# A fused attention, dense and expert kernel: TensorE's order inside an expert tile

## The reference

```python
# x: 3072 x 512 (output of the dense layer), w1: 8 x 512 x 1024, w2: 8 x 1024 x 512
logits = x @ w_gate
expert_idx = np.argmax(logits, axis=1)
probs = softmax(logits)
gate_w = probs[np.arange(N), expert_idx]
for e in range(8):
    mask = expert_idx == e
    h = np.maximum(x[mask] @ w1[e], 0.0)
    out[mask] = gate_w[mask, None] * (h @ w2[e])
```

## Time and profile before

| | |
|---|---|
| median of 3 runs | 1019.3 us |
| profiled execution | 1019.65 us |
| its span | 1017.9 us |
| TensorE matmuls busy | 987.9 us (97%) |
| TensorE weight loads busy | 854.0 us (84%) |
| VectorE busy | 505.1 us (50%) |
| ScalarE busy | 431.8 us (42%) |
| GpSimd busy | 158.5 us (16%) |
| mean granted TensorE clock | 0.995 of full speed |

### The profile page before, as it was taken

The page is one execution under the profiler, slowest core; times in us unless marked ns, Lnnn a source line. Parts: engine busy times, 40 slices in busy tenths (PEclk is TensorE's granted clock), DMA queues, the critical chain, the costliest instruction groups (busy, mean ns, idle before and its releaser), DMA issues.

```text
span 1017.9 us, 17631 instructions
## 1 busy us (share of the span) xinstructions
PE 987.9 (97%) x5968; PEld 854.0 (84%) x5969; DVE 505.1 (50%) x1003; ACT 431.8 (42%) x756; POOL 158.5 (16%) x171
## 2 busy tenths in 40 slices
PE   6999999999999999999999999999999999999995
PEld 5888888888888888888888988888888888888873
DVE  3553455455465366366365587563223423335553
ACT  2755444444544444444444546333223323335541
POOL 3020100011011011011010002121222222233330
PEclk9999999999999999999999999999999999999998
DMA  8433211111111121121020014155111311451830
GB/s 327 145 147 124 73 42 43 61 55 42 53 63 42 42 74 42 35 81 43 27 84 5 32 42 145 52 201 213 42 49 34 116 54 42 193 209 60 336 129 11
DMA packets 28774, 91.83 MB, mean 90 GB/s; under 512 B 4062, under 2 KB 4190, under 8 KB 23584
## 3 DMA queue, kind: packets, MB, share of 16 engines
q1 hardware_dynamic: 23904, 76.48, 21.2%
q0 software_dynamic: 4800, 14.42, 4.4%
HBM read 78.30 MB, written 13.89 MB: 91 GB/s over the span
## 4 chain that ended last, share of the span: by engine, by line
PE 90%; DVE 3%; issue 3%; ACT 1%; DMA 1%; DVEq 1%; ACTq 0%; SPq 0%; POOL 0%; POOLq 0%
PE ps L1356 26%; PE ps L1339 25%; PE ps L1470 15%; PE ps L1445 13%; PE ps L1252 3%; PE ps L1260 2%; PE ps L1455 2%; PE ps L1277 1%; PE ps L1429 1%; PE ps L1269 1%; DMA arena<-qT 1%; DMA arena<-x_rows,arena 1%; ACT W L692 0%; DVEq L1189 0%; DVE W L1073 0%
## 5 line engine op out<-in xcount | busy, mean ns | idle before, releaser
L1356 PE MATMUL ps<-W,GS 128*128 128x512 f32 x1152 | 292.0, 397 | 3.2 <-DVE GS L847 3.2
L1339 PE MATMUL ps<-XS,W 128*128 128x384 f32 x1536 | 289.9, 337 | 1.6 <-DVE XS L810 1.6
L1339 PEld LDWEIGHTS ps<-XS,W 128*128 128x128 f32 x1536 | 272.4, 188 | 12.8 <-DVE XS L810 1.8
L1356 PEld LDWEIGHTS ps<-W,GS 128*128 128x128 f32 x1152 | 211.2, 188 | 49.5 <-issue 4.2
L1470 PE MATMUL ps<-W,XS 128*128 (+1 forms) x696 | 167.2, 396 | 6.7 <-DVE XS L1083 6.7
L1445 PE MATMUL ps<-W,XS 128*128 (+1 forms) x696 | 170.6, 394 | 0.0
L1470 PEld LDWEIGHTS ps<-W,XS 128*128 128x128 f32 x696 | 129.6, 189 | 34.2 <-issue 8.3
L638 ACT ACTIVATE arena<-ps 128x384 f32<-128x384 f32 x128 | 62.8, 491 | 222.3 <-PE ps L1339 216.4
L1445 PEld LDWEIGHTS ps<-W,XS 128*128 128x128 f32 x696 | 128.4, 188 | 25.6 <-DVE XS L1077 0.3
L843 DVE SCALAR_TENSOR_TENSOR arena<-ps,arena 128x384 f32<-128x384 f32 x128 | 71.1, 555 | 130.7 <-ACT arena L642 130.7
L858 DVE CUSTOM_DVE_ANT_0 arena<-arena 128x512 bf16<-128x512 f32 x168 | 127.0, 794 | 0.0
(11 more groups left out here) (167 smaller groups left out, 652.7 us busy)
## 6 DMA issues: line engine op xcount, KB each, us to landing
arena<-w SPq DMA_DIRECT2D x32, 1024.0 KB, 6.8
arena<-kT SPq DMA_DIRECT2D x24, 256.0 KB, 2.8
arena<-qT SPq DMA_DIRECT2D x24, 256.0 KB, 3.3
arena<-v SPq DMA_DIRECT2D x24, 256.0 KB, 4.0
arena<-k SPq DMA_DIRECT2D x24, 256.0 KB, 4.2
x_rows<-arena SPq DMA_DIRECT2D x24, 256.0 KB, 4.8
arena<-w_out SPq DMA_DIRECT2D x4, 1024.0 KB, 5.0
arena<-w_in SPq DMA_DIRECT2D x3, 1024.0 KB, 4.9
```

The source lines that it names most:

```text
L1339: last = pe.matmul(ps_h[g % 2], w_in_s[a][:, g // 4, k_, (g % 4) * P:(g % 4 + 1) * P], xs[half][b][:, k_, :], start=(k_ == 0 and a + b == ...
L1356: last = pe.matmul(ps_x[s], GS[:, g % 2, a, s * P:(s + 1) * P], w_out_s[b][:, g, :], start=(g == 0 and a + b == 0), stop=(g == GF - 1 and ...
```

## The change

In `tile` the h transposes come first, the x transposes right behind them, then one `steer` and both halves of `mm1` of the next tile, then `steer` and `mm2`. The same is done to the written-out tile 3. The written-out tiles 0 to 2, all other engines' programs, and the work itself stay as they are.

```diff
             def tile(j, q, arrived, ahead=2):
-                if ahead >= 1:
-                    nvisit, npar = steer(j + 1)
-                    mm1(j + 1, 0, nvisit, npar)
                 h_transpose(j, ahead == 0)
-                if ahead >= 1:
-                    mm1(j + 1, 1, nvisit, npar)
                 if ahead >= 2:
                     x_transpose(j + 2, q, arrived)
+                if ahead >= 1:
+                    visit, par = steer(j + 1)
+                    mm1(j + 1, 0, visit, par)
+                    mm1(j + 1, 1, visit, par)
                 visit, par = steer(j)
                 mm2(j, visit, par)
...
+            h_transpose(3)
+            x_transpose(5, 1, 48)
             mm1(4, 0, 0, 0)
-            h_transpose(3)
             mm1(4, 1, 0, 0)
-            x_transpose(5, 1, 48)
             mm2(3, 0, 0)
```

## The result

The changed kernel is slower: 1029.98 us (median of 6 runs, 1027.05 to 1033.05) against 1019.57 us for the kernel before (6 runs, 1017.49 to 1022.61). The ratio is 1.0096, 95% interval 1.0075 to 1.0118. The profiled execution took 1030.56 us, its span is 1028.8 us. The forecast was 1019.8 us, no change, in a range to 1024. The kernel is 10 us slower than that, 6 us beyond the range's end.

A forecast was written before the change was run, and what follows sets the result against it. It took the expert stage to be bound by TensorE; terms of 0, 0, -0.7, +1.2, 0 and 0 summed to +0.5 us, on the median 1019.3 + 0.5 = 1019.8 us, no change, range 1015.8 to 1024.

The forecast's parts named there:

- (a): TensorE, fewer changes between transposes and matmuls: a tile stays at 12.24 us, value 0, within 0.75 us either way.
- (b): Wait of `mm2` for `h_low` in w1 refill tiles: unchanged, as VectorE is in the w1 pieces; value 0.
- R1: Rival: earlier h transposes remove the waits for `h_low` except the last tile's, 5.5 us, giving 1013.8 us; chance 0.05.
- (c): ScalarE's chain with a w2 refill: the w2 piece starts 0.35 us sooner in two tiles, value -0.7 us.
- (d): Gather read earlier by the x transposes: waits of 0.8 and 0.4 us in two tiles, +1.2 us, bounds 0 and +4.
- (e): The two `steer`: loads ahead of `mm1` need 1.8 us, hidden under 2.15 us of queued work; value 0, at most +0.4.
- R2: Rival: `steer` ahead of `mm1` lies open in each of 24 tiles, 16 us in all, 46 without cover; chance 0.07.
- (f): The last `mm2`, partly at half clock, 7.2 us: value 0, bounds -1.7 and 0.
- R3: Rival: transposes without matmuls lower the clock, 40 us in 24 tiles, 3.3 in the two with gather wait; chance 0.03.

The follow-up runs named there:

- h_only: Changed kernel with only the h transposes moved, the x transposes put back between `mm1` and `mm2`: 1019.98 us, ratio 0.999 to the kernel before.
- after_again: The changed kernel itself, unedited, run again on another chip: 1027.3 us, ratio 1.0082 to the kernel before.
- steer_first: Changed kernel with the `steer` ahead of `mm1` moved ahead of the h transposes: 1023.53 us, ratio 1.0033 to the kernel before.
- gather_early: Changed kernel with GpSimd issuing each gather one tile earlier, ahead of the scatter: 1022.05 us, ratio 1.0005 to the kernel before.
- waits_swapped: Changed kernel with an extra, long fulfilled wait ahead of the gather's, to put the latter on the first transpose's weight load: 1027.86 us, ratio 1.008.
- double_steer: Changed kernel with the `steer` ahead of `mm1` done twice behind the transposes: 1050.09 us, ratio 1.0294 to the kernel before.

## Why the prediction was wrong

(a) held: 12.23 us from `mm2` to `mm2`, against 12.24.

(b) held, and R1 with its 0.05 is refuted: the row for L1083 has 6.1 us where it had 6.7, and h_only has 6.3.

(c) was worth 0, not -0.7. `mm2` to `mm2` with both refills is 14.23 us (975.57 to 989.80), before 14.22. ScalarE in that tile:

```profile
975.77 0.60 ACT L704 ACTIVATE arena<-ps 128x512 f32<-128x512 f32 x1 [2.12 <-PE ps L1445]
976.26 0.59 ACT L698 ACTIVATE XS<-ps 128x512 fp32r<-128x512 f32 x1
977.20 7.33 ACT L692 ACTIVATE W<-arena 128x2048 f32 x4 [0.34 <-issue]
```

The gap ahead of the w2 piece did shrink, from 0.70 to 0.34 us. But `relu` begins 0.20 us behind the start of `mm2`, where it began 0.16 us ahead of it. The prediction had this right, and it takes away what the gap gives: the piece still starts 1.63 us after `mm2` (977.20 - 975.57), exactly as in the earlier trace rows. The sum from `mm2` on in the prediction, 1.3 us, needed a gap of zero, and 0.34 us of it stay though nothing seen in the trace is waited for.

(d) named the right cause, the right row and two of the four tiles, the others being among those that it called possible, and its size lay in the bounds of 0 to 4: the x transposes start 2.8 us late in four tiles, 1.1 us at most. The 1.2 us that went into the sum were less than half of it, since only those two were counted.

(e) is the step that failed, in the sentence "the sequencer runs 16 pairs of load and matmul ahead". That holds while nothing ahead of it is missing. I had read it from one tile without a late input and then applied it to tiles for which (d) had just forecast a missing one. The sequencer is then not 16 pairs ahead but at the x transposes, and what stands behind them in program order, `steer` with 1.8 us, begins with the landing. The cost of a late gather is its wait plus 1.45 us. It even comes without a wait: since `steer` can't begin before the landing and needs 1.8 us, a gather that lands less than about 1.4 us ahead of the x transposes already makes `mm1` late (by 0.3 us twice in the changed kernel, by 1.46 us at 798 in after_again). That is R2's mechanism ("fewer than about 14 pairs ahead"), but in four tiles, not 24; I had worked it out only for all or none. It is shown by steer_first (the loads moved, the gather still late), by gather_early (the gather moved, the loads still there) and by waits_swapped.

The cover in undisturbed tiles was also read too small, 2.15 us where 2.57 was measured, which cost nothing.

(f) and R3: the last `mm2` took 7.3 us, before 7.2. The half clock came, in two tiles and for 3.2 us, as R3 had it for "the two with the wait" (3.3 us). I gave it almost nothing since I took the stretch to be 2.1 us; with the open `steer` it was 3.65 and 3.78.

The terms as measured are 0 (a), 0 (b), 0 (c), +2.8 (d), +5.7 (e), +3.2 (R3). With them the forecast would have been some 1031 us. (The lower end of the stated range, 1015.8, is 0.3 below what its own bounds give, 1019.3 - 3.2 = 1016.1; nothing hangs on it.)

## What to carry to other kernels

When a new wait goes in ahead of instructions that run in a sequencer (register loads, address work, branches), price it as the wait plus all of those, since the lead that hides them is gone at that moment, and ask for data that is early by their length and not merely in time; put such loads ahead of the wait. A cover measured in an undisturbed stretch is no cover in the tiles where something is late, and two small costs in the same tile can bring a third, here the clock. Moving a consumer earlier needs its producer moved as well: the same new order on TensorE costs 1% with the old gathers and nothing with earlier ones.

## What the runs showed of the hardware

- In these runs TensorE's sequencer came to the loads of `steer` only when the gather had landed, whether the wait was on an instruction of its own (changed kernel, 915.0) or on the weight load of a transpose (waits_swapped, 873.5): 4.5 us "issue" in 4 waits in both.
- The clock did not fall by the length of a stretch without large matmuls alone. In the changed kernel it fell after 3.65 and 3.78 us with twelve transposes in them and not after 3.00. In waits_swapped, with the same matmuls and transposes in that tile and the same DMA share, it did not fall after 3.64:

```profile
871.66:875.30 3.64, 1.69 (x13) 1.22 (x12) 1.95 (x3) 1.09 (x2) 1.40 (x3) 1.00 1.00 391
875.30:880.85 5.55, 5.55 (x25) 4.65 (x25) 0.09 (x1) 0.60 (x1) 1.05 (x1) 1.00 0.46 168
```

- It fell also in double_steer after 3.96 us (801.21 to 805.17) with a DMA share of 0.00, where the two above had 1.00 and 0.99, so the clock can fall there without transfers:

```profile
801.21:805.17 3.96, 1.48 (x14) 1.24 (x12) 2.04 (x3) 1.09 (x2) 1.40 (x3) 1.00 0.00 1
805.17:812.34 7.17, 7.17 (x24) 5.78 (x25) 0.00 (x0) 0.60 (x1) 1.05 (x1) 0.76 0.16 45
```

- But in gather_early one `mm2` ran at half clock after a plain standstill of 1.86 us, while the 2.34 us of the earlier trace rows and the 1.46 us ahead of 989.80 left the clock alone. What decides it stays open:

```profile
977.99:979.85 1.86, 0.01 (x1) 0.00 (x1) 1.86 (x3) 1.08 (x2) 1.86 (x1) 1.00 0.37 154
979.85:987.02 7.17, 7.17 (x25) 5.71 (x26) 0.93 (x2) 0.00 (x0) 1.28 (x3) 0.76 0.22 77
```
